# Scaled r and k of a pair in one five-part tile, and a fourth first-layer matrix loaded in round 3

## The reference, cut to what matters

```
for t in range(S):
    cur = einsum('bhd,bhe->bhde', u * kt, vt)
    y[:, :, t] = einsum('bhd,bhde->bhe', rt, state + cur)
    state = wt * state + einsum('bhd,bhe->bhde', kt, vt)
```

## Time and profile before

| | us |
|---|---|
| median of three runs | 556.15 |
| profiled execution, own time | 555.19 |
| its span on the core | 553.4 |
| TensorE busy in matmuls | 485.5 (88%) |
| VectorE busy | 334.6 (60%) |
| ScalarE busy | 332.8 (60%) |
| GpSimd busy | 13.7 (2%) |

### The profile page before, as it was taken

How to read it: one execution, slowest core, us unless ns; L and a number is a source line. 1 busy time by engine, 2 the same in 40 slices (tenths; PEclk the granted TensorE clock), 3 DMA queues, 4 the chain that set the end, 5 groups by cost and what they waited for, 6 DMA issues and landing times.

```text
span 553.4 us, 18757 instructions
## 1 busy us (share of the span) xinstructions
PE 485.5 (88%) x7850; PEld 425.1 (77%) x7850; DVE 334.6 (60%) x583; ACT 332.8 (60%) x689; POOL 13.7 (2%) x21
## 2 busy tenths in 40 slices
PE   1778889798989898678698879999999999999996
PEld 0557768677777777667333469999999999999996
DVE  5688868587878788925341167555555555555552
ACT  1787677686868687434221276656565656565653
POOL 9000000000000000000000000000000000000000
PEclk9998989798989899959889979999999999999999
DMA  6885565736262621293799730101010101010101
GB/s 112 146 213 103 150 113 152 137 70 117 57 118 52 114 56 34 59 403 136 238 390 369 260 114 1 44 1 44 1 43 2 43 0 43 0 43 1 44 1 43
DMA packets 119788, 56.23 MB, mean 102 GB/s; under 512 B 102944, under 2 KB 116256, under 8 KB 119328
## 3 DMA queue, kind: packets, MB, share of 16 engines
q1 hardware_dynamic: 116512, 42.54, 31.1%
q10 hardware_dynamic: 3200, 12.58, 6.1%
HBM read 50.38 MB, written 4.72 MB: 100 GB/s over the span
## 4 chain that ended last, share of the span: by engine, by line
PE 72%; ACT 11%; issue 7%; SPq 4%; DVE 4%; DMA 0%; ACTq 0%; DVEq 0%
PE bank L707 12%; PE bank L708 12%; PE bank L709 12%; ACT wide L802 4%; PE ybank L485 4%; PE lbank L468 4%; PE ybank L501 4%; PE lbank L451 4%; PE bank L697 4%; SPq L289 4%; PE tbank L402 3%; PE tbank L415 2%; PE bank L646 2%; PE bank L623 2%; ACT wl L743 2%
## 5 line engine op out<-in xcount | busy, mean ns | idle before, releaser
L707 PE MATMUL bank<-wo_high,h_high 128*128 128x384 f32 x384 | 129.6, 337 | 1.8 <-DVE h_low L1207 1.6
L708 PE MATMUL bank<-wo_low,h_high 128*128 128x384 f32 x384 | 129.0, 336 | 0.0
L709 PE MATMUL bank<-wo_high,h_low 128*128 128x384 f32 x384 | 128.9, 336 | 0.0
L953 ACT ACTIVATE h_relu<-bank 128x384 f32<-128x384 f32 x128 | 62.9, 492 | 74.4 <-PE bank L697 74.1
L1205 DVE CAST h_high<-h_sq 128x384 fp32r<-128x384 f32 x128 | 46.0, 359 | 96.7 <-PE bank L709 88.0
L1041 DVE TENSOR_TENSOR rk<-rk,wl 112x768 f32<-112x768 f32 x80 | 76.3, 954 | 36.7 <-PE lbank L468 19.9
L707 PEld LDWEIGHTS bank<-wo_high,h_high 128*128 128x128 f32 x384 | 72.6, 189 | 3.2 <-issue 2.7
L1207 DVE TENSOR_TENSOR h_low<-h_sq,h_high 128x384 fp32r<-128x384 f32 x128 | 71.5, 558 | 4.5
L708 PEld LDWEIGHTS bank<-wo_low,h_high 128*128 128x128 f32 x384 | 72.7, 189 | 0.0
L709 PEld LDWEIGHTS bank<-wo_high,h_low 128*128 128x128 f32 x384 | 72.5, 189 | 0.0
L957 ACT ACTIVATE h_sq<-h_relu 128x384 f32<-128x384 f32 x128 | 67.4, 527 | 4.1
(11 more groups left out here) (123 smaller groups left out, 532.5 us busy)
## 6 DMA issues: line engine op xcount, KB each, us to landing
w_sb<-in_moe_w_dram ACTq DMA_DIRECT2D x8, 1536.0 KB, 8.7
w_hi<-in_moe_w_dram SPq DMA_DIRECT2D x16, 384.0 KB, 8.0
nat<-in_w_dram SPq DMA_DIRECT2D x64, 72.0 KB, 2.4
nat<-in_r_dram SPq DMA_DIRECT2D x64, 72.0 KB, 2.5
nat<-in_k_dram SPq DMA_DIRECT2D x64, 72.0 KB, 2.4
v_tok<-in_v_dram SPq DMA_DIRECT2D x32, 144.0 KB, 3.1
w_lo<-in_moe_w_dram SPq DMA_DIRECT2D x1, 4608.0 KB, 16.8
out_dram<-o_sb SPq DMA_DIRECT2D x8, 576.0 KB, 3.0
```

What stands on the lines that cost most here:

```text
L707: nc.tensor.matmul(acc, hi, wo_high[:, fb, :], start=(fb == 0), stop=False)
L708: nc.tensor.matmul(acc, hi, wo_low[:, fb, :], start=False, stop=False)
L709: last = nc.tensor.matmul(acc, lo, wo_high[:, fb, :], start=False, stop=(fb == NF - 1))
L953: nc.scalar.activation(h_relu[fb % 2][:], h_bank[fb % 2][:, 0:GT * P], ACT.Relu).then_inc(relu_done, 1)
```

## The change

The three tiles `[P, 2, S]` of a pair become one tile `[P, 5, S]`. Parts 0 to 2 hold the scaled r of three rounds in turn (through `R_SLOT`), parts 3 and 4 the scaled k of two. `rk_at(rd, s, x)` picks the part. `scaled_half`, the operand of L1041, takes the distance of the two parts into its stride; at level 0 it reads `rt` and writes `rk` as before. GpSimd has six memsets in place of ten, and ScalarE waits for the first four. `W1_EARLY` is 4: matrix 3 is loaded in round 3, in the middle of round 7 two are left (4 and 5), and ahead of the last two at the end ScalarE's queue waits for the last update of both pairs and for the last copies of w into `w_scan`.

```diff
-    W1_EARLY = 3
+    W1_EARLY = 4
+    R_SLOT = (0, 2, 1)
...
-        rk2 = [sb(f"rk2_{s}", [P, 2, S], c=att) for s in range(2)]
-        rk0 = [sb(f"rk0_{s}", [P, 2, S], c=att) for s in range(2)]
...
-        rk1 = [sb(f"rk1_{s}", [P, 2, S], c=att) for s in range(2)]
+        rk = [sb(f"rk{s}", [P, 5, S], c=att) for s in range(2)]
...
+        def rk_at(rd, s, x):
+            return rk[s][:, 3 + rd % 2 if x else R_SLOT[rd % 3], :]
+
-        def scaled_half(tile, m):
+        def scaled_half(tile, m, first=0, second=1):
             at = tile[:]
-            return bass.AP(at.tensor, at.offset + m, [[at.ap[0][0], 112], [S - m, 2], [2 * m, S // (2 * m)], [1, m]])
+            return bass.AP(at.tensor, at.offset + first * S + m,
+                           [[at.ap[0][0], 112], [(second - first) * S - m, 2], [2 * m, S // (2 * m)], [1, m]])
...
-            for n, tile in enumerate(rt + rk0 + rk1 + rk2 + wide):
+            for n, tile in enumerate(rt + rk + wide):
                 if n:
                     pool.wait_ge(rows_zero, n)
-                pool.memset(tile[96:P] if n < 8 else tile[:], 0.0).then_inc(rows_zero, 1)
+                pool.memset(tile[96:P] if n < 4 else tile[:], 0.0).then_inc(rows_zero, 1)
...
-            act.wait_ge(rows_zero, 8)
+            act.wait_ge(rows_zero, 4)
             inputs_out(0, 0, 12)
-            act.wait_ge(rows_zero, 10)
+            act.wait_ge(rows_zero, 6)
...
                 if rd == ROUNDS - 1:
+                    for s in range(2):
+                        act.wait_ge(updated[s], 6 * ROUNDS)
+                        act.wait_ge(w_spread[s], ROUNDS)
                     load_w1(act, NE - 2, NE)
...
-                nc.vector.tensor_tensor(scaled_half(rk[rd % 3][s], m), scaled_half(rk[rd % 3][s] if lv else rt[s], m), by,
+                out = scaled_half(rk[s], m, R_SLOT[rd % 3], 3 + rd % 2)
+                nc.vector.tensor_tensor(out, out if lv else scaled_half(rt[s], m), by,
                                         ALU.mult).then_inc(updated[s], 1)
```

More of the change, by code:

```diff
@@ L118, in fused_kernel @@
         w_scan = [sb(f"w_scan{s}", [P, D, NC], c=att) for s in range(2)]
-        rk, aa = (rk0, rk1, rk2), (aa0, aa1)
+        aa = (aa0, aa1)
         att.close()
@@ L414, in turn_k @@
                         t0 = (3 * g + i) * P
-                        last = nc.tensor.transpose(bank[:, i * 112:(i + 1) * 112], rk[rd % 3][s][0:112, 1, t0:t0 + P],
+                        last = nc.tensor.transpose(bank[:, i * 112:(i + 1) * 112], rk_at(rd, s, 1)[0:112, t0:t0 + P],
                                                    ident[0:112, 0:112])
@@ L444, in level @@
                     pe.wait_ge(updated[s], 6 * rd + lv)
-                src = rt[s] if lv == 0 else rk[rd % 3][s]
+                right, left = ((rt[s][:, 0, :], rt[s][:, 1, :]) if lv == 0 else
+                               (rk_at(rd, s, 0), rk_at(rd, s, 1)))
                 if lv in WIDE:
@@ L450, in level @@
                         dst = lbank[s][C * par:C * par + C, 0:2 * PER * SUB].rearrange("p (h x) -> p h x", h=2)
-                        last = nc.tensor.matmul(dst[:, :, SUB * i:SUB * i + SUB], src[:, 1, C * c:C * c + C],
+                        last = nc.tensor.matmul(dst[:, :, SUB * i:SUB * i + SUB], left[:, C * c:C * c + C],
                                                 wide[s][:, :, SUB * c:SUB * c + SUB], start=True, stop=True)
@@ L463, in level @@
                         dst = lbank[s][C * par:C * par + rows, at:at + width]
-                        mov = src[a:b, 0, t0:t0 + C]
+                        mov = right[a:b, t0:t0 + C]
                         if lv:
@@ L467, in level @@
                             mov = mov.rearrange("p (n two m) -> p n two m", two=2, m=m)[:, :, 1, :]
-                        last = nc.tensor.matmul(dst, src[a:b, 1, t0:t0 + rows], mov, start=True, stop=True)
+                        last = nc.tensor.matmul(dst, left[a:b, t0:t0 + rows], mov, start=True, stop=True)
                 last.then_inc(level_mm[s], 1)
@@ L500, in y_far @@
                             at = 512 * h + i * D
-                            last = nc.tensor.matmul(ybank[rows, at:at + D], rk[rd % 3][s][a:b, 0, C * c:C * c + C],
+                            last = nc.tensor.matmul(ybank[rows, at:at + D], rk_at(rd, s, 0)[a:b, C * c:C * c + C],
                                                     kv[s][a:b, :, c], start=False, stop=(i == PER - 1),
@@ L761, in input_out @@
                 if with_u:
-                    evac(use, rk[rd % 3][s][0:112, x, half::2], src)
+                    evac(use, rk_at(rd, s, x)[0:112, half::2], src)
             def inputs_out(rd, first, count):
@@ L800, in widen @@
                 for h, (a, b) in enumerate(HEADS):
-                    right = rk[rd % 3][s][a:b, 0, :].rearrange("p (n two m) -> p n two m", two=2, m=m)[:, :, 1, :]
+                    right = rk_at(rd, s, 0)[a:b].rearrange("p (n two m) -> p n two m", two=2, m=m)[:, :, 1, :]
                     nc.scalar.activation(wide[s][a:b, h, :].rearrange("p (n m) -> p n m", m=m), right, ACT.Copy)\
```

## The result

The changed kernel has a median of 558.04 us over 20 runs (554.28 to 561.54), the kernel before 555.03 over 20 (552.13 to 557.36). The ratio is 1.0058, with a 95% interval of 1.0037 to 1.0079: 3.2 us slower. A second comparison, on another occasion (experiment 5), gave 1.0034 (1.0011 to 1.0058), 1.9 us. All ratios leave out the slow runs, which lie over 1.5% above the fastest of their kernel. The profiled execution has 557.78 us and a span of 556.0, 2.6 us longer than before.

What follows compares the result with a forecast made beforehand. TensorE, 72% of the chain, was taken as the bound; 0 + 1.4 + 0 + 1.0 + 0 = +2.4 us gave 557.6 on the profiled 555.19 and 558.5 on the median 556.15. Forecast 558.0, range 553 to 561.5.

Steps and rivals of the forecast that it cites:

- Nothing waits for w1: Expert stage: the first expert product is released by VectorE, not a DMA, so an earlier fourth matrix gains nothing by arriving.
- Start, 0: Kernel start: the gain from fewer memsets is hidden by SyncE's busy queue, the cover; 0, bounds 0 and -1.4 us.
- Rival E: Expert stage: the fourth early matrix lets it start sooner; 0 us, 2% together with anything else.
- Rival C: Kernel start: the memset gain is real, 1.4 us off, giving 556.2 us; chance 10%.
- Round 3, +1.4: Second `y_far` of round 3: the new load delays the instruction fetch, stop grows by 2.9, +1.4 us stays; bounds 0, +2.9.
- The absorption: After round 3's stop: VectorE and ScalarE catch up while TensorE stands, so only +1.4 of 2.9 us stays.
- Rival D: Round 3: the whole stop stays, +2.9, half clock behind it +2.5, then 1.0: +6.4, 561.6 to 562.5 us; chance 11%.
- Round 7's load, 0: Middle of round 7: two matrices instead of three leave TensorE's 3.10 us stop as it was; 0, bounds 0 and -2.8.
- Rival B: Round 7: the stop goes, -2.8 us, and a higher clock saves 2.9; -3.3 in all, 552.0 to 552.8 us; chance 10%.
- The wait at the end, +1.0: End of round 7: ScalarE's last two load issues come later, delaying the `k_tok` copies; +1.0 us, bounds +0.4 and +1.5.
- Strides, 0: L1041: other distances between its parts cost nothing; 0, bounds 1 us to either side.

Runs made afterwards that it cites:

- experiment 5: The changed kernel, unaltered, timed once more beside the kernel before: 557.62 us, ratio 1.0034.
- experiment 9: The changed kernel with no w1 load before round 7 and all eight matrices on SyncE's queue: 550.61 us, 0.9926 to the kernel before.
- experiment 4: The changed kernel with the first four v loads and the phi load issued behind round 1's r, k and w: 558.36 us, 1.0022 to the kernel before.
- 3: The changed kernel with the last two w1 loads and their waits moved from ScalarE's to SyncE's queue: 556.52 us, 1.0010 to the kernel before.
- 8: The changed kernel with matrix 3 loaded again in rounds 4, 5 and 6: 567.10 us, 1.0202 to the kernel before.
- 1: The changed kernel with matrix 3 loaded in round 7 again and no load in round 3: 557.29 us, 1.0019 to the kernel before.
- 2: The kernel before with only the four new waits ahead of the last two loads: 557.12 us, 1.0014 to the kernel before.
- 11: The kernel before, its six tiles kept, with all w1 loads from round 7 on SyncE's queue: 550.38 us, 0.9896 to the kernel before.
- 12: The changed tiles, all w1 loads in round 7 on SyncE's queue, first v and phi loads behind round 1's r, k, w: 550.61 us, 0.9898.
- experiment 6: The changed kernel with matrix 3 loaded some 8 us earlier in round 3, in a quiet stretch: 559.53 us, 1.0060 to the kernel before.
- experiment 10: The changed kernel with each early matrix in three 512 KB DMAs and the last two matrices on SyncE's queue: 552.13 us, 0.9945.

## Why the prediction was right

I said 558.0, the median is 558.04. Part of that is luck: I added 2.4 us to numbers (555.19 and 556.15) that were above the 20-run median of the kernel before, 555.03. The change itself is 3.2 us in one comparison and 1.9 in the other, around my 2.4.

- *Nothing waits for w1*: right in every profile; with matrices 0 to 3 loaded some 90 to 175 us later (experiment 9) it is still right. Rival E falls.
- *Start, 0*: right, 0.24 us came through, and experiment 4 shows the cover. Rival C falls. The wait for the DMA that I had put at over 1 us was 0.73 in this profile and 1.83 in experiment 5.
- *Round 3, +1.4*: the mechanism is right to its numbers (issue 2.05 us behind the first `y_far`, forecast 2.0 to 2.3; on again 8.9 us behind the issue, forecast 8.7; a stop of 3.19, forecast 3.2). The size was too small. In the two profiles the stretch grew by 1.66. But over five profiles with the load (changed kernel 30.11, and 30.21, 30.08, 29.50, 29.93 in experiments 5, 3, 4, 8) it is 30.0 us in the mean, and over six without (28.45 before, and 27.34, 27.48, 26.99, 27.00, 27.54 in 1, 2, 9, 11, 12) 27.5: 2.5 us (2.7 without the kernel before's own 28.45). The absorption that I read out of 20.4 against 19.0 is not there: from the end of the stop to the next first `y_far` pass 19.1 to 19.4 us in the five profiles with the load and 18.8 to 18.9 in five of the six without. My 20.4 was the sixth, in which the clock was granted at 0.56 and 0.58 from 133 to 137 us. The stop is 3.0 us in the mean with the load and 0.55 without, so all of the difference stays. And the clock falls behind the stop in all five profiles with the load, in none of the other five without. From 134 to 136 us, the changed kernel and then experiment 1, the clock third from the end:

```profile
134.00:136.00 2.00, 2.00 (x93) 1.82 (x81) 1.37 (x2) 1.95 (x5) 0.00 (x0) 0.52 0.64 117
134.00:136.00 2.00, 1.54 (x42) 1.29 (x34) 1.02 (x1) 1.66 (x5) 0.00 (x0) 1.00 0.81 135
```

Rival D is right that the stop stays; of its 2.5 us for the clock behind it some 0.3 came (19.2 us from the stop on against 18.9, where it asked for over 20.4).

- *Round 7's load, 0*: right, 3.31 against 3.10 us. Rival B falls for two matrices. Over more profiles the stop with three matrices was 3.10, 2.70 (experiment 2) and 1.38 (experiment 1), and with two 2.39 to 3.58 in seven (the changed kernel and experiments 3 to 6, 8 and 10): with two it is 0.8 us longer in the mean, and three profiles are too few to say whether that is the change's. That fewer bytes in flight do help is seen in rounds 1 and 2 of experiment 10.
- *The wait at the end, +1.0*: right; +1.33 in the profile, where the two issues took 1.17 us instead of 0.92, and +1.08 in experiment 2 by itself. (The sum should start at 243.40, the end of the update: 244.41, not 244.45. Likewise rival B's -3.3 us give 551.9.)
- *Strides, 0*: right; the update takes 952 ns in place and 954 from `rt` in the changed kernel, against 954 and 956.

With 2.5 for round 3, 1.1 for the wait and 0.2 off for the start the terms make 3.4 us, near the first comparison's 3.2 and just above the upper end of the second (3.2). The rule of the Trainium skill's page "Runtime: NRT & Kernel Launch" ("Instruction fetch mechanics"), that crossing a block is mostly hidden, holds here only while no 1536 KB load is in flight: 0.15 to 0.9 us a stop in the second `y_far` of rounds 1 to 3 in experiments 9, 11 and 12, against 2.4 to 3.6 with one.

What is open: why the fetch waits for most of a load. No run moved the instruction stream against the loads with everything else equal, and none takes out round 3's load and the wait at the end together and leaves the rest.

## What to carry to other kernels

Before an early load is called free, look at what the engine with the longest list does while it is in flight: idle time put down to "issue" that moves by a fixed number of instructions each round points to the instruction stream, and each large transfer beside it cost 2.5 to 3.2 us here. Load late, where the list is sparse and just before the need, or try small pieces and look where their stops fall (in experiment 10 they helped in rounds 1 and 2 and not in round 3), and keep waits with their issues on a queue that has nothing behind them. When a stretch is read from one profile, look at its granted clock first.

## What the hardware showed that I had not expected

- A stop of 1.75 us ahead of dense matmuls cost more than one of 3.19 us behind them; the clock stayed at 1.2 GHz from 124 to some 134 us behind it (experiment 6), and from 122 to 134 us behind one of 1.22 us (experiment 10).
- GpSimd's memset of 32 partitions took 1.37 us for 1536 elements and 3.3 for 3840 (6.64 for two): 2.4 times the time for 2.5 times the elements, so nearly all of it goes by size.
- Two DMA issues on ScalarE's queue took 0.92 us in most profiles, 1.17 and 1.37 in the two of the changed kernel, and its activations behind them waited for them.
